# Reading the 512 columns of both products last to first, with the weight buffers set 128 bytes off them

## The reference

```python
w = np.exp(weight_gen - np.max(weight_gen, axis=-1, keepdims=True))
w = w / (np.sum(w, axis=-1, keepdims=True) + 1e-09)
x_pad = np.concatenate([np.zeros((B, K - 1, D)), x], axis=1)
x_unf = x_pad[:, idx, :].reshape(B, S, K, H, group)
out = np.einsum('bshk,bskhg->bshg', w, x_unf)

h = x @ w_in                               # 16384 x 192 by 192 x 2048
g = h * (1.0 / (1.0 + np.exp(-1.702 * h)))
return g @ w_out                           # 2048 x 192
```

## Time and profile before

| | |
|---|---|
| median of 3 runs | 1129.38 us (1128.94 to 1129.43) |
| the profiled execution, its own time | 1129.01 us |
| its span, first to last instruction | 1127.2 us |
| TensorE, matmul | 1113.8 us busy, 99% of the span, 9748 instructions |
| TensorE, weight loads | 914.3 us, 81%, 9748 instructions |
| VectorE | 803.6 us, 71% |
| ScalarE | 620.5 us, 55% |
| GpSimd | 7.9 us, 1% |
| DMA | 38 GB/s over the span |

### The profile page before, as it was taken

How to read it: one execution, slowest core, us unless ns; L and a number is a source line. 1 busy time by engine, 2 the same in 40 slices (tenths; PEclk the granted TensorE clock), 3 DMA queues, 4 the chain that set the end, 5 groups by cost and what they waited for, 6 DMA issues and landing times.

```text
span 1127.2 us, 21689 instructions
## 1 busy us (share of the span) xinstructions
PE 1113.8 (99%) x9748; PEld 914.3 (81%) x9748; DVE 803.6 (71%) x714; ACT 620.5 (55%) x655; POOL 7.9 (1%) x9
## 2 busy tenths in 40 slices
PE   7999999999999999999999999999999999999998
PEld 4788878888888888888888888888888888888886
DVE  7998988677576866759667596775867757686322
ACT  6676655565554646455464555545556555454543
POOL 2000000000000000000000000000000000000000
PEclk9999999999999999999999999999999999999999
DMA  8601010101001010010100101001010100100000
GB/s 274 218 7 53 15 53 2 39 29 40 29 1 40 29 40 29 1 40 29 40 29 1 65 4 40 29 22 46 1 40 29 40 29 1 40 29 1 29 1 29
DMA packets 8892, 42.68 MB, mean 38 GB/s; under 512 B 1056, under 2 KB 1312, under 8 KB 6496
## 3 DMA queue, kind: packets, MB, share of 16 engines
q1 hardware_dynamic: 8400, 40.51, 10.9%
q0 software_dynamic: 400, 0.79, 0.4%
HBM read 24.77 MB, written 12.58 MB: 33 GB/s over the span
## 4 chain that ended last, share of the span: by engine, by line
PE 94%; DVE 4%; ACT 1%; DMA 0%; issue 0%; ACTq 0%; DVEq 0%; SPq 0%
PE hid L630 45%; PE acc_main L646 30%; PE acc_rest L646 20%; DVE conv L393 1%; DVE gate_lo L548 1%; DVE prod L386 1%; DMA gate<-in_x_first 0%; ACT gate_hi L313 0%; ACT gate L310 0%; DVE hid L469 0%; DVE w L441 0%; DVE prod L411 0%; DVE prod L463 0%; ACT L255 0%; ACT L310 0%
## 5 line engine op out<-in xcount | busy, mean ns | idle before, releaser
L310 ACT ACTIVATE gate<-hid 128x1024 f32<-128x1024 f32 x256 | 263.1, 1028 | 464.6 <-PE hid L630 463.9
L548 DVE TENSOR_TENSOR gate_lo<-gate,gate_hi 128x1024 fp32r<-128x1024 f32 x256 | 311.5, 1221 | 258.0 <-ACT gate_hi L313 258.0
L630 PE MATMUL hid<-xt,w_hi 64*128 64x512 f32 x3072 | 431.8, 387 | 0.0
L630 PEld LDWEIGHTS hid<-xt,w_hi 64*128 64x128 f32 x3072 | 287.4, 184 | 62.7 <-ACT gate_hi L313 2.1
L646 PE MATMUL acc_main<-gate_hi,w 64*128 64x512 f32 x2048 | 315.8, 386 | 0.7 <-DVE gate_lo L548 0.7
L313 ACT ACTIVATE gate_hi<-hid 128x1024 fp32r<-128x1024 f32 x256 | 261.1, 1020 | 0.0
L646 PEld LDWEIGHTS acc_main<-gate_hi,w 64*128 64x128 f32 x2048 | 191.5, 184 | 42.0 <-DVE gate_lo L548 1.7
L630 PE MATMUL hid<-xt,w_lo 64*128 64x512 f32 x1536 | 215.8, 386 | 0.0
L646 PE MATMUL acc_main<-gate_lo,w 64*128 64x512 f32 x1024 | 199.4, 386 | 0.0
L646 PE MATMUL acc_rest<-gate_hi,w 64*128 64x512 f32 x1024 | 199.4, 386 | 0.0
L646 PE MATMUL acc_rest<-gate_lo,w 64*128 64x512 f32 x1024 | 199.4, 386 | 0.0
(11 more groups left out here) (54 smaller groups left out, 228.1 us busy)
## 6 DMA issues: line engine op xcount, KB each, us to landing
xwin<-in_x_runs SPq DMA_DIRECT2D x15, 1056.0 KB, 4.9
out<-outs_main SPq DMA_DIRECT2D x13, 512.0 KB, 2.6
out<-outs_rest SPq DMA_DIRECT2D x13, 256.0 KB, 2.9
taps<-in_tap_runs SPq DMA_DIRECT2D x1, 3136.0 KB, 10.0
taps<-in_w_rows SPq DMA_DIRECT2D x2, 1536.0 KB, 9.8
w_hi<-w_hi SPq DMA_DIRECT2D x2, 768.0 KB, 9.5
w_lo<-w_lo SPq DMA_DIRECT2D x2, 768.0 KB, 7.2
out<-outs_main SPq DMA_DIRECT2D x6, 256.0 KB, 2.1
```

Source lines behind the costliest of these rows:

```text
L310: nc.scalar.activation(gate[:, v % 2, :, :], hid[:, v % 2, :, :], ACT.Gelu_apprx_sigmoid).then_inc(gate_ready, 1)
L548: nc.vector.tensor_tensor(gate_lo[:, v % SLOTS, :, :], gate[:, v % 2, :, :], gate_hi[:, v % SLOTS, :, :], ALU.subtract).then_inc(gate_lo_r ...
L630: last = nc.tensor.matmul(hid[:, v % 2, h, :], w[rows, k if j else slice_of(h, k), q, f], xt[rows, j % 2, part, k, :], start=(i == 0), sto ...
```

## The change

Two things. First, the three weight buffers are allocated 256 bytes larger, and the weights lie from byte 128 of each on (`sb_on`, `ON = 32` elements). Everything behind them moves up by whole multiples of 256 bytes: `xt` begins at 149632, `gate_hi` at 182400, `gate_lo` at 198784, all three still 128 past a multiple of 256, while the weights now begin at multiples of 256 (16640, 41472, 66304). Second, each matmul of both products reads its 512 columns with step -1 (`BACK`). The first product thus writes `hid` with its tokens in reversed order, `gate`, `gate_hi` and `gate_lo` hold them reversed, and the second product's reversed reading puts them right again in `acc_main` and `acc_rest`. Each engine's instructions and waits stand in the same order as before; none is added and none goes.

```diff
+ON = 32
...
-        w1_hi = sb("w1_hi", [P, SLICES, 2, FH], F32R)
-        w1_lo = sb("w1_lo", [P, SLICES, 2, FH], F32R)
-
-        w2 = sb("w2", [P, CH, 2 * D], F32R)
+        def sb_on(name, pattern, n, **sizes):
+
+            return sb(name, [P, n + HALF], F32R)[:, ON:ON + n].rearrange(pattern, **sizes)
+
+
+        w1_hi = sb_on("w1_hi", "p (k q f) -> p k q f", SLICES * 2 * FH, k=SLICES, q=2)
+        w1_lo = sb_on("w1_lo", "p (k q f) -> p k q f", SLICES * 2 * FH, k=SLICES, q=2)
+
+        w2 = sb_on("w2", "p (c d) -> p c d", CH * 2 * D, c=CH)
...
+            BACK = slice(None, None, -1)
+
             def first_product(j, v):
...
-                                                xt[rows, j % 2, part, k, :], start=(i == 0), stop=(i == len(terms) - 1))
+                                                xt[rows, j % 2, part, k, BACK], start=(i == 0), stop=(i == len(terms) - 1))
...
-                        done = nc.tensor.matmul(acc[:, h, :], w2[rows, chunk[h], cols], g[rows, s, h, :],
+                        done = nc.tensor.matmul(acc[:, h, :], w2[rows, chunk[h], cols], g[rows, s, h, BACK],
                                                 start=start, stop=stop)
```

## The result

The changed kernel takes **1159.87 us** (median of 4 runs, 1159.77 to 1160.05); the kernel before, run beside it, 1129.31 us. The ratio is 1.0272, with a 95% interval from 1.0259 to 1.0285: it is slower by 30.6 us. The prediction of 1084 us, and its range up to 1140 us, were wrong. The way that it went is rival B.

What follows compares the result with a forecast made beforehand. TensorE's distance between matmul pairs was taken as the bound. At 9.7 ns less a pair, 41 us after 161 us and 4 us before it made 45 us, so 1129.0 became 1084 us; range 1072 to 1140 us.

Steps and rivals of the forecast that it cites:

- rival B: All matmul pairs: the two reads settle worse with columns reversed, 5.0 ns more a pair, about 1154 us; chance 0.14.
- What bounds the kernel: TensorE, 99% busy with matmuls: time is the number of pairs times the distance between their starts, 226.7 ns.
- The excess of 13.3 ns: Each of 4864 pairs takes 13.3 ns more than its columns' 213.3 ns, 64.7 us in all; read as clashing reads.
- the likeliest single outcome is that nearly all of it goes: Offset and direction together remove most of each pair's excess: 217 ns a pair, 9.7 ns less; chance 0.40.
- 231.7 ns right after a wait: Six pairs after TensorE's wait at 56 us stand 231.7 ns apart, not 226.7; taken as sign that reads clash.
- Rival A: All matmul pairs: the 13.3 ns depend on neither address nor direction, so nothing changes, 1129 us; chance 0.20.
- Rival C: Column reads with step -1 cost two cycles each: 426.7 ns a pair, about 2100 us; chance 0.08.
- Rival D: All matmul pairs: only part of the clash goes, 219 to 225 ns a pair, 1092 to 1121 us; chance 0.18.
- The covers: Other engines' work beside TensorE: after 161 us nothing new becomes late, VectorE going from 68% to 72% in wide pieces.
- the worry about VectorE: First 161 us: VectorE, 91% busy, would deliver some `gate_lo` late, TensorE waiting 1 to 3 us; 4 of 6 us counted.

## Why the prediction was wrong

**What bounds the kernel.** Right, and it stayed so: the time went with the distance between pairs to within about a microsecond (32 us against 31.1), and nothing else became late.

**The excess of 13.3 ns depends on where the reads stand to each other.** Right in kind. The offset alone moved the rate from 226.5 to 232.2 ns, and with standing columns the pair took 216 ns: some 11 of the 13 ns go when the columns stand still or walk at half the pace. The rest is there in every run. The 215.7 ns of the Trainium skill ("TensorE: Matmul & The Clock Gate", Part 1), which I had set beside the trace, is what the runs with repeated columns give.

**The step that failed** is "the likeliest single outcome is that nearly all of it goes", from which I took 217 ns a pair. I had treated the excess as a clash that one avoids by moving the streams apart. Moving them apart did not remove it: the pair took 233.2 ns, 6.6 more than before where I had counted on 9.7 less. The runs showed a stream of pairs that holds one of several rates, which I read as repeating patterns, and among the nine kernels in which all 128 weights and all 512 columns were read, the pattern of 226.7 ns was the lowest. It came only with upward columns, and steadily only with weights at the same place modulo 256 bytes (the kernel before, the padded version, the version shifted as a whole); at 16 bytes it was met in some executions. The kernel before stood in the best pattern seen, and each move away from it that was tried kept or lost it. I had a sign of this in hand: 231.7 ns right after a wait against 226.7 long after the earlier trace rows. I read it as a sign of a clash. It could as well be read so that 226.7 was the settled, favourable case.

**Rival B** named this mechanism and was given 0.14. Its reason, a step that repeats and is lost, fits what the runs show, but it put the loss on the direction alone, and the offset alone cost 26 us too. Its price was too small: 5.0 ns a pair by the six pairs after a wait, 6.6 measured, so 1154 us instead of 1160. The range was cut through the middle of this rival, at 1140 us. Having a row of this very kernel at 231.7 ns, I should have given that rate more weight than a value under 226 which no row showed.

**Rival A** fell: the offset of the weights alone cost 26 us. The Trainium skill ("TensorE: Matmul & The Clock Gate", Part 2) has two independent read ports for columns and weights, and speaks for this rival; here the measurement decides, and the rate does depend on where the weights stand. **Rival C** fell too; reading backward at full rate costs 7 ns a pair, not 200. **Rival D** fell: no run of the real product showed a gain.

**The covers.** VectorE and ScalarE never came into play, since TensorE got slower. The runs at 216 ns show that the worry about VectorE was just, and that I had it too small. The waits of the run with one column address:

```profile
ACT gate L315 <- PE hid L638: 391.3, 204, 2.5
...
PEld acc_main L654 <- DVE gate_lo L553: 11.0, 18, 1.6
```

Of these 11.0 us, 5.4 lie before 161 us, where I had expected 1 to 3, and 5.6 behind it, in 12 waits, where I had written that nothing becomes late. The kernel before waits 1.7 us in all there. With them the gain of that run is 42 us, and not the 52 us that 4864 pairs at 10.7 ns less would give.

**What stays open.** Why 226.7 ns is left is not shown, nor what a column read at full speed meets. That the weight loads take part is shown by the offset alone. That fewer weights left 226.7 ns as it was speaks against a simple count of meetings. A matmul without a load of its own beside it was not tried, because each of these matmuls brings its load; and not every offset was tried, so that a pattern below 226.7 ns may exist.

## What to carry to other kernels

Where TensorE is full, divide a long stretch by the number of matmuls before any edit: the distance over the pure column time is the most that can be won, and here it moved with the relative addresses of weights and columns: 64 bytes between them cost 2.7%, so that a new buffer of an odd size may do so too, while one of 256 bytes cost nothing. If the settled rate is better than the one right after a wait, as here, take it for a sign that the layout is already in a favourable pattern; each change of direction or offset tried here kept or lost it, and none improved on it. Try such offsets one at a time and in several executions, since the same addresses can settle in two ways.

## What the runs showed of the hardware that I had not expected

- fp32r matmuls of 512 walking columns stand 226.7 to 235 ns apart, with each column read twice, or one column all the time, 216 ns, at the same granted clock; one matmul on 64 rows costs as much as two side by side.
- One kernel (weights 16 bytes off) takes 1130 or 1159 us from execution to execution, and in one execution went from 233 to 226.7 ns a pair at a wait of 0.38 us.
- A change between 128-row and 64-row matmuls costs 0.21 us each time (227.8 us in 1077 changes); the weight loads are idle for 0.30 us at it.
